# Attention in nine query tiles per pair of heads, with an fp32 product with V and the third transpose round behind the next scores

## The reference

```python
q_pool = q.reshape(B, H, S // 2, 2, D).mean(axis=3)      # 576 queries of 64 per head
scores = q_pool @ k.T / 8;  scores -= scores.max(-1)      # 576 x 1152
attn = exp(scores) / (exp(scores).sum(-1) + 1e-9)
x = heads side by side of (attn @ v)                      # 1152 tokens x 512
x = sum_e p[:, e] * (relu(x @ w1[e]) @ w2[e])             # 4 experts, all tokens
out = gate * (relu(x[m] @ v1[e]) @ v2[e])                 # 8 experts, each token one
```

## Time and profile before

| what | us |
|---|---|
| median of 3 runs (lowest to highest) | 1003.75 (1002.01 to 1004.75) |
| span of the profiled execution | 1002.8 |
| PE busy in it | 879.9 (88%) |
| DVE, ACT, POOL busy | 511.9, 435.0, 285.1 |
| mean granted clock of PE | 0.972 |

### The profile page before, as it was taken

How to read it: one execution, slowest core, us unless ns; L and a number is a source line. 1 busy time by engine, 2 the same in 40 slices (tenths; PEclk the granted TensorE clock), 3 DMA queues, 4 the chain that set the end, 5 groups by cost and what they waited for, 6 DMA issues and landing times.

```text
span 1002.8 us, 14755 instructions
## 1 busy us (share of the span) xinstructions
PE 879.9 (88%) x4740; PEld 753.5 (75%) x4741; DVE 511.9 (51%) x901; ACT 435.0 (43%) x794; POOL 285.1 (28%) x166
## 2 busy tenths in 40 slices
PE   2888888888888879999999999999999709999996
PEld 2666666666666768898989898989898607878885
DVE  4788888888878854141414141314131322299225
ACT  4677777777777643030303031303131502278224
POOL 3766667766667521000000000000000040133112
PEclk9999999999999979999999999999999858999998
DMA  8333222234227221010201120012000062197510
GB/s 263 83 83 84 71 59 59 59 81 95 59 59 185 75 85 52 33 49 37 84 1 32 53 84 0 22 62 84 1 1 1 0 235 70 42 308 255 209 42 23
DMA packets 30095, 79.66 MB, mean 79 GB/s; under 512 B 4008, under 2 KB 4008, under 8 KB 30065
## 3 DMA queue, kind: packets, MB, share of 16 engines
q1 hardware_dynamic: 27104, 70.58, 23.9%
q0 software_dynamic: 2960, 8.68, 2.7%
HBM read 69.52 MB, written 10.78 MB: 80 GB/s over the span
## 4 chain that ended last, share of the span: by engine, by line
PE 76%; ACT 7%; issue 6%; DVE 6%; DMA 3%; POOL 1%; SPq 1%; ACTq 0%; POOLq 0%; DVEq 0%
PE L L337 20%; PE L L400 20%; PE ring L322 7%; PE L L505 7%; PE L L479 6%; PE ring L309 4%; PE scores L290 4%; PE scores L291 3%; ACT a L550 2%; DVE aTl L700 2%; ACT aTh L514 2%; PE ring L307 1%; DMA xr<-sorted_rows 1%; ACT o_vl L514 1%; POOL sorted_rows L1069 1%
## 5 line engine op out<-in xcount | busy, mean ns | idle before, releaser
L1021 POOL TENSOR_TENSOR a<-a,rinv 128x1152 f32<-128x1152 f32 (+1 forms) x80 | 168.5, 2106 | 106.2 <-DVE rinv L754 104.1
L700 DVE TENSOR_TENSOR aTl<-ring,aTh 128x384 fp32r<-128x384 f32 (+1 forms) x240 | 118.5, 512 | 62.0 <-ACT aTh L514 60.6
L309 PE MATMUL ring<-ident,a 128*128 128x128 f32 (+1 forms) x672 | 110.4, 277 | 37.1 <-ACT o_vl L514 18.2
L514 ACT ACTIVATE aTh<-ring 128x384 fp32r<-128x384 f32 (+1 forms) x240 | 106.5, 458 | 70.9 <-PE ring L309 66.3
L619 ACT ACTIVATE hh<-L 128x384 fp32r<-128x384 f32 x96 | 46.6, 491 | 204.2 <-PE L L337 204.2
L337 PE MATMUL L<-xTh,w1h 128*128 128x384 f32 x384 | 131.2, 342 | 4.4 <-DVE hl L832 2.3
L337 PE MATMUL L<-xTl,w1h 128*128 128x384 f32 x384 | 130.8, 341 | 0.0
L337 PE MATMUL L<-xTh,w1l 128*128 128x384 f32 x384 | 130.6, 340 | 0.0
L1069 POOL DMA_INDIRECT sorted_rows<-acc,posi x9 | 10.7, 1186 | 415.0 <-DVE posi L924 412.6
L309 PEld LDWEIGHTS ring<-ident,a 128*128 128x128 f32 (+1 forms) x672 | 75.4, 145 | 64.9 <-DVE aTl L700 32.8
L832 DVE SCALAR_TENSOR_TENSOR hl<-L,hh 128x384 fp32r<-128x384 f32 x96 | 52.8, 557 | 125.4 <-ACT hh L619 125.4
(11 more groups left out here) (155 smaller groups left out, 1580.6 us busy)
## 6 DMA issues: line engine op xcount, KB each, us to landing
raw<-in_v SPq DMA_DIRECT2D x48, 512.0 KB, 5.9
raw<-in_w SPq DMA_DIRECT2D x32, 512.0 KB, 5.2
rawK<-in_kT SPq DMA_DIRECT2D x32, 288.0 KB, 5.1
rawQ<-in_qT SPq DMA_DIRECT2D x32, 288.0 KB, 5.8
sorted_rows<-filler SPq DMA_DIRECT2D x19, 257.0 KB, 9.4
rawV<-in_vr SPq DMA_DIRECT2D x16, 288.0 KB, 5.9
xr<-sorted_rows POOLq DMA_DIRECT2D x15, 257.0 KB, 3.0
out<-o,destc POOLq DMA_INDIRECT x13, 2.8
```

What stands on the lines that cost most here:

```text
L309: last = pe.transpose(o, src, ident[0:m, 0:m])
L514: return act.activation(o, i, ACT.Copy, **kw)
L700: return dve.tensor_tensor(o, i0, i1, op)
L1021: pool.tensor_tensor(a[t][0:m, :], a[t][0:m, :], rinv[0:m, t:t + 1].to_broadcast([m, SEQ]), ALU.mult).then_inc(S["norm_ready"], 1)
```

## The change

The experts' code stays. In the attention:

- **Nine tiles per pair.** Each head has four full tiles; the last 64 queries of both heads form one shared tile (index 4, `XT`). Its scores are 12 matmuls of 384 columns instead of 6: the operand of each head is padded with zeros to 128 columns.
- **No hi/lo split of the exp result.** The ring is copied once as fp32 into `aT`: round 0 by ACT, rounds 1 and 2 by DVE. Three exp buffers instead of five.
- **Product with V in fp32**, twice per pair: for each of 9 key tiles two matmuls with 64 weight columns (V of the head), one for each 288 queries, whose results go to partitions 0 to 63 and 64 to 127 of one bank.
- **Normalization after the product.** DVE takes 1/sum once per pair, POOL spreads it (`spread`), PE turns it with five transposes through the ring ("N" turns, after tiles 2 and 3 of the next pair), and DVE multiplies it on the way from o to y. POOL no longer touches the exp result.
- **Preparing K and Q** moves from ACT and DVE to POOL, except for the first head; the split of x moves to POOL too, except for the last pair.
- **Order on PE**: transposes 0 and 1 of tile g, scores of tile g + 3, transposes 2, then V (after tiles 5 and 0) and N.
- **Loads**: V of a head is loaded apart from K and Q, after the earlier product; the loop over pairs is unrolled.

```diff
-QT = [(t * P, min(P, QS - t * P)) for t in range(-(-QS // P))]
-TPP = 2 * TPH
-V_TILES = (3, 0)
-S_LEAD, E_LEAD, N_LEAD = 4, 3, 2
+TPP = 2 * FULL + 1        # 9
+XT = FULL                 # 4: the shared tile
+HALF = QS // 2
+LEAD = 3
+V_STEP = (5, TPP)
+N_STEP = (2, 3)
...
@@ SP @@
+            for n in range(2, NH):
+                s = n % 2
+                sp.wait_ge(S["k_lo"], n - 1)
+                sp.wait_ge(S["q_sum"], n - 1)
+                load_kq(n, s)
+                sp.wait_ge(S["o_ready"], n - 1)
+                load_v(n, s)
@@ PE @@
+            def score_part(g, chunks):
...
+                if chunks[0] == 0 and (k == 0 or k == XT):
+                    pe.wait_ge(S["k_lo"], 2 * j + (k == XT) + 1)
+                    pe.wait_ge(S["q_lo"], 2 * j + (k == XT) + 1)
+                if chunks[0] == 0:
+                    at_least(pe, S["exp_ready"], g - 1)
+                heads = ((0, X_COLS[0]), (1, X_COLS[1])) if k == XT else \
+                    ((tile_head(k)[0], q_cols(*tile_head(k))),)
...
+            def times_v(j, s):
+                newest = TPP * j + (XT, TPP - 1)[s] + 1
+                for r in range(RPT):
+                    pe.wait_ge(S[f"a_out{r}"], newest)
+                pe.wait_ge(S[f"v_in{s}"], 16 * (j + 1))
+                turn = ("V", j, s)
+                bank_free(pe, turn)
                 for kt in range(KT_N):
+                    for u in range(2):
+                        last = pe.matmul(bank(turn)[u * DH:(u + 1) * DH, 0:HALF], V[s][:, kt, :],
+                                         aT[:, kt, s, u * HALF:(u + 1) * HALF],
+                                         start=(kt == 0), stop=(kt == KT_N - 1))
                 last.then_inc(S["o_ready"], 1)
...
+            for g in range(LEAD):
+                score_part(g, range(SC))
+            for g in range(TPP * PAIRS):
+                j, k = g // TPP, g % TPP
+                transpose_round(g, 0)
+                transpose_round(g, 1)
+                if g + LEAD < TPP * PAIRS:
+                    score_part(g + LEAD, range(SC))
+                transpose_round(g, 2)
+                for s, when in enumerate(V_STEP):
+                    if when % TPP == k and j >= when // TPP:
+                        times_v(j - when // TPP, s)
+                if k in N_STEP and j:
+                    spread_rinv(j - 1, N_STEP.index(k))
+            for f in range(2):
+                up_tile(0, 0, f)
+            times_v(PAIRS - 1, 1)
+            spread_rinv(PAIRS - 1, 0)
+            spread_rinv(PAIRS - 1, 1)
+            for f in range(2, L1_BANKS):
+                up_tile(0, 0, f)
@@ ACT, tile g @@
+                        take_o(j - (when + 1) // TPP, s)      # tiles 6 and 1: partitions 0 to 63 of V's bank
+                take_a(g)                                     # round 0
+                if g + 2 < TPP * PAIRS:
+                    exp_tile(g + 2)
@@ DVE, tile g @@
+                if g + 2 < TPP * PAIRS:
+                    max_tile(g + 2)
...
+                        take_o(j - (when + 1) // TPP, s)      # the other half
+                if k - 1 in N_STEP and j:
+                    normalize(j - 1, N_STEP.index(k - 1))
+                take_a(g, 1)
+                take_a(g, 2)
+                if k == TPP - 1:
+                    rinv_pair(j)
@@ POOL @@
+            def prep_k(n, s):
+                p = n // 2
+                at_least(pool, S["s_ready"], (TPP * (p - 1) + (XT + 1, TPP)[s]) if p else 0)
+                pool.wait_ge(S[f"kq_in{s}"], 64 * (p + 1))
+                pool.tensor_copy(KT[s][:], rawK[s][:]).then_inc(S["k_hi"], 1)
...                                                           # lo half, 64 x 1152
+            def prep_q(n, s):                                 # add, scale, copy (hi), subtract (lo), each 128 x 576
...
+            prep_k(1, 1)
+            prep_q(1, 1)
+            for j in range(PAIRS):
+                if j:
+                    spread_pair(j - 1)
+                if j + 1 < PAIRS:
+                    prep_k(2 * j + 2, 0)
+                    prep_q(2 * j + 2, 0)
+                if j:
+                    split_x(j - 1)
+                if j + 1 < PAIRS:
+                    prep_k(2 * j + 3, 1)
+                    prep_q(2 * j + 3, 1)
+            spread_pair(PAIRS - 1)
```

More of the change, by code:

```diff
@@ L203, in bank_free, with tile_head @@
[L203 to L212, removed]
+        def tile_head(k):
+            return (0, k) if k < XT else (1, k - XT - 1)
@@ L294, in transpose_round @@
-            def transpose_round(t, k, r, j, g, first):
-                m = QT[t][1]
+            def score_part(g, chunks):
+                j, k = g // TPP, g % TPP
+                if g == XT and chunks[0] == 0:
+                    pe.wait_ge(S["pads_ready"], 4)
+                if chunks[0] == 0 and (k == 0 or k == XT):
[5 more added lines that the diff above has]
+                    ((tile_head(k)[0], q_cols(*tile_head(k))),)
+                for c in chunks:
+                    keys = slice(c * SW, (c + 1) * SW)
+                    n = 0
+                    for s, cols in heads:
+                        for Q in (QTh, QTl):
+                            last = pe.matmul(scores[g % 2][:, c, 0:SW], Q[s][:, cols], KT[s][:, keys],
+                                             start=(n == 0), stop=(n == 2 * len(heads) - 1))
+                            n += 1
+                    if c == SC - 1:
+                        last.then_inc(S["s_ready"], 1)
@@ L297, in transpose_round @@
+            def transpose_round(g, r):
                 if r == 0:
-                    pe.wait_ge(S["norm_ready"], g + 1)
-                bank_free(pe, j, ("T", k, r), first)
+                    pe.wait_ge(S["exp_ready"], g + 1)
+                turn = ("T", g, r)
+                bank_free(pe, turn)
                 for i in range(KPR):
                     kt = KPR * r + i
-                    o = bank(("T", k, r))[:, i * m:(i + 1) * m]
-                    src = a[t][0:m, kt * P:(kt + 1) * P]
-                    if m < P and i == 0:
-                        last = pe.matmul(o, src, ident[0:m, 0:m], start=True, stop=True)
-                    else:
-                        last = pe.transpose(o, src, ident[0:m, 0:m])
@@ L310, in transpose_round @@
-                last.then_inc(S["t_ready"], 1)
-            def times_v(n, s, u, j, k, first=False, very_last=False):
-                q0, w = PVG[u]
-                pe.wait_ge(S["a_lo"], RPT * (TPH * n + (V_TILES[0], TPH)[u]))
-                pe.wait_ge(S["v_lo"], n + 1)
-                if not very_last:
-                    bank_free(pe, j, ("V", k, u), first)
-                O = bank(("V", k, u))
+                    last = pe.transpose(bank(turn)[:, i * P:(i + 1) * P], a[g % 3][:, kt * P:(kt + 1) * P], ident[:])
@@ L324, in times_v, with spread_rinv @@
                 last.then_inc(S["o_ready"], 1)
+            def spread_rinv(j, part):
+                pe.wait_ge(S["spread_ready"], 2 * (j + 1))
+                turn = ("N", j, part)
+                bank_free(pe, turn)
+                for i, t in enumerate((range(FULL), (XT,))[part]):
+                    last = pe.transpose(bank(turn)[:, i * P:(i + 1) * P], spread[:, t * P:(t + 1) * P], ident[:])
+                last.then_inc(S["nb_ready"], 1)
             def up_tile(e, c, f):
```

442 lines of the change are left out of this document (175 added, 267 removed).

## The result

| | before | after |
|---|---|---|
| median of 4 runs each, same chip (us) | 1003.33 (1002.01 to 1004.75) | 972.73 (968.56 to 974.02) |
| span of the profiled execution | 1002.8 | 971.4 |
| pair to pair (before: a steady pair, after: mean of 7) | 42.78 | 40.5 |
| fifth expert tile starts | 384.01 | 350.98 |
| mean granted clock of PE | 0.972 | 0.962 |

The ratio is 0.9689, with a 95% interval of 0.9667 to 0.9711: 31 us faster, where 52 were forecast. The profiled execution took 973.05.

The account below looks back on a forecast made before the run. A chain through several engines, no single one, was taken to set the 42.78 us pair. Pairs of 38.3 us plus start and end put the fifth expert tile at 332.4 instead of 384.01: gain 51.6, predicted 952, range 928 to 1018.

Parts of the forecast that it names:

- V side by side: Product with V on PE: the two 64-column matmuls of a key tile run concurrently, 4.54 us per V; chance 0.58.
- one after the other: Rival in V's 36 instructions: halves run in sequence, 9.07 us per V, 1013 us in all; chance 0.21.
- The loop: Plain tile: DVE's copy of round 2, PE's round 1 and scores, then round 2; 2.60 us per tile.
- The tiles after the N turns: Tiles 3 and 4: round 1 waits for DVE's maximum and multiplication, 1.8 and 1.6 us late, 3.4 per pair.
- POOL: Second head's K and Q, loaded after V, are ready at 17.6 but wanted at 16.0: PE waits 1.6 us per pair.
- A pair then takes 38.3: Steady attention pair: 36.7 us from V steps, plain tiles, shared tile, normalization and 1/sum, plus PE's 1.6 us wait for POOL.
- hidden better: Rival on normalization and POOL: without their 3.4 and 1.6 us per pair, 917 us; chance 0.05.
- the start: Start of attention: scores at 14.3, transposes at 21.2, 23.0 in effect after waiting for the second head's K and Q.

Follow-up runs that it names:

- e1: Changed kernel with V's two loops swapped, all nine key tiles of one query half, then of the other: 1005.98 us, ratio 1.0005 to the kernel before.
- e3: Changed kernel with SP's queue reordered, the next K and Q loaded as soon as their buffer is free, ahead of V: 951.26 us, ratio 0.9456.
- e5: Changed kernel with fourteen extra identity transposes just before PE's wait for POOL ahead of the shared tile: 966.28 us, ratio 0.9617.
- e4: Changed kernel with eight extra identity transposes ahead of round 0 of tiles 3 and 4, filling the holes after the N turns: 972.36 us, ratio 0.9668.
- e10: e3 (early loads) with V's two loops swapped as in e1: 1006.38 us, ratio 1.0014, 55.1 us over e3.
- e11: e3 in which ACT also copies rounds 1 and 2 out of the ring and DVE copies them only after it: 994.62 us, ratio 0.99.
- e9: e3 with normalization before the maximum (e7) and all three transpose rounds ahead of the scores: 929.09 us, ratio 0.9257.
- e7: e3 with DVE doing the normalization of tiles 3 and 4 before the maximum instead of behind it: 931.40 us, ratio 0.9263.
- e2: Changed kernel without normalization: no N turns, DVE copies o to y instead of multiplying: 951.19 us, ratio 0.9459.

## Why the prediction was right, and what it missed

**V side by side: right, and all depended on it.** Forecast 4.54, measured 4.52. The view of a window of 0.3 us shows it: the instructions that run in the window are six within 0.90 us in the kernel after, and three within 0.91 in e1.

```profile
158.75 0.90 PE L353 MATMUL ring<-aT,V 128*64 128x288 f32 x6
```

```profile
146.66 0.91 PE L353 MATMUL ring<-aT,V 128*64 128x288 f32 x3 [0.29 <-DVE aT L738]
```

The price of one instruction was 0.252 and is 0.243, 2 cycles per column. The Trainium skill (TensorE: Matmul & The Clock Gate, "Part 3: Packing small matmuls — row/col tiling") has distinct column groups run concurrently; these runs agree, with 7.94 / 4.52 = 1.76 times for two halves of 64.

**The rival "one after the other" had the wrong size**: 7.94 us instead of 9.07, because some instructions around the change of half run in twos. With such a V the prediction's own sum gives 952 + 54.7 - 11.2 = 995.5, just faster than before; measured are 1006.0, no change (1.0005). The 10 us between are not V's: e1 has neither a wait for POOL nor a fall of the clock in its pairs, and these take 43.93, 0.4 more than the sum has, 3 us in seven; the others lie before and behind them.

**The loop: right.** 2.58 for 2.60 a plain tile. From a pair's first product to its second 15.06 to 15.19 us for 15.0 (V, 3.15, two plain tiles, 0.3 and 1.79). The tiles after the N turns are late by 1.85 and 1.64 (143.74, 148.17 and 152.39 are one point of three neighbouring tiles, with 2.58 taken off each step) for 1.8 and 1.6.

**POOL: right in place and size, by two errors that cancel.** K and Q are there 8.5 us after the product's end (122.45 to 130.96), not 7.5; POOL needs 9.4 for a head (130.96 to 140.32), not 10.1: 17.9 for 17.6. PE is ready for them 16.3 us after that end (140.43 less the hole of 1.64), not 16.0. PE waits 1.8 us a pair (1.57 to 2.29), forecast 1.6. That the sum came out is in part luck.

**What failed: the step from there to a pair.** "A pair then takes 38.3" took every hole for its own length. The pairs took 40.5. The two in which the clock held took 38.98 and 39.00, close to the forecast; the five in which it fell for 3.4 or 6.8 us took 1.1 to 3.1 more, 10.4 together (0.6 of it is the longest wait for POOL, 2.29, in the pair from 158.21). e3 and e5 show that without the holes ahead of the shared tile the falls are gone from all these pairs but the last of e3; e4, which fills the other holes instead, keeps five of them. Nothing in the prediction stood for it, although its rows had a stretch at 0.50 and its sum had the holes of 1.6 us and of the N turns.

The Trainium skill warns in the same page (TensorE: Matmul & The Clock Gate, "Why this matters for your kernels") of idle gaps of PE between bursts of matmuls, which bring its clock down. The trace agrees in kind but not in size: the gaps that the page warns of are longer than any here, and the clock fell with holes of at most 2.29 us.

**The sum, in spans.** Forecast 951.2, measured 971.4, 20.2 more: seven pairs, 15.2 (283.3 instead of 268.1: 10.4 in the pairs with falls of the clock; 2 because the wait for POOL is 1.9 instead of 1.6 a pair; 3 because the rest of the pair is 37.1 instead of 36.7); from the last pair's first product to the fifth expert tile 28.85 instead of 25.2, 3.6 (PE waits 2.5 for the experts' first weights on DVE, and the clock falls again); the experts 620.4 instead of 618.8, 1.6; the start -0.3 (scores at 13.49, transposes at 20.64). e3's steady pairs, with neither POOL's wait nor a fall of the clock, take 37.1 where the prediction has 36.7 before POOL. So half of the 20 us is the clock, for which the prediction had no term, and the rest is small terms.

**The rival "hidden better" (917)** pointed at the two terms that were there to be had: with the loads early and the multiplication first, the runs give 931.

**Open.** Why the clock falls in some pairs and not in others with the same holes: the pair from 199.3 has a hole of 1.65 us ahead of the shared tile and no fall, that from 117.9 one of 1.64 and a fall; e3's last pair and one of e10 have a fall without a wait for POOL. In e11, without that wait but with holes of 0.8 us at the plain tiles, six of the seven pairs have one or two. No single hole decides, and what PE's standing still must add up to is not shown. Why e9 gains so little over e7; that its loop of scores, maximum and exp is next is only argued.

## What to carry to other kernels

Price a hole in a busy PE at more than its length: where the granted clock fell, the pair lost 1 to 3 us more, so the cheapest hole to remove may be a load that stands in SP's queue behind one that must wait. If a bank in PSUM goes round PE and two other engines, ask first for one reader, and then what the next engine has to do. Two matmuls of 64 columns that write different partition halves are to be written alternately: the same work, one half after the other, gave the whole gain back.

## What the runs showed of the hardware

- **An fp32 matmul with 64 weight columns and 288 moving ones** is two instructions of 0.243 us. Two such on different column halves start 0.01 us apart and take 0.243 together.
- **The halves overlap for a while even when written one after the other.** In e1 eight instructions around the change of half still start in twos (the steps there are 0.01 to 0.06 and 0.19 to 0.24, elsewhere 0.24); that is the 0.8 us between 36 x 0.243 = 8.75 and 7.94. If two instructions of one half never overlap, which the even 0.24 elsewhere suggests, some of the second half must have started ahead of the last of the first. The rows don't say which half an instruction belongs to, so this stays an inference.
- **DVE's copy within SBUF can wait for POOL.** A copy of 128 x 512 fp32 took 0.42 us in e2 when it started first, and 2.77 when it started 0.15 us after a POOL subtraction of 2.63; it ended 0.29 after that. The subtraction beside the 0.42 took 2.93. The changed kernel's multiplication at that place reads PSUM and takes 0.68.
- **Dead work can make a program faster.** Fourteen transposes of the identity in a hole kept the granted clock at 1.00 in the seven pairs, and 972.7 became 966.3.
- **POOL prices**: the fp32r copy of 128 x 1152 takes 1.15 us, where a multiplication of that size took 2.11; the 128 x 576 operations 1.40 (add, subtract), 1.65 (scale), 0.66 (copy).
